# Plain float32 products for the DFTs, folds in place on VectorE, and the second sequence's transforms placed inside the first MoE

## What is computed

```python
batch, seq, dim = (2, 3008, 256)
X = np.fft.fft(x, axis=1)
X = np.fft.fft(X, axis=2).real          # attn_out
h = x @ w_in                            # 6016 x 256 @ 256 x 2048
g = h * (1.0 / (1.0 + np.exp(-h)))
x = g @ w_out
h = x @ w_in2
g = np.maximum(h, 0.0) + alpha * np.minimum(h, 0.0)
out = g @ w_out2
```

## Time and profile before

| | us |
|---|---|
| median of 3 runs | 1013.82 |
| lowest and highest | 1011.83, 1015.05 |
| the profiled execution, its own time | 1014.12 |
| its span, first to last instruction | 1012.3 |
| PE busy (4268 matmuls) | 969.5 |
| ACT, POOL, DVE busy | 590.4, 531.4, 452.8 |

### The profile page before, as it was taken

The page is one execution under the profiler, slowest core; times in us unless marked ns, Lnnn a source line. Parts: engine busy times, 40 slices in busy tenths (PEclk is TensorE's granted clock), DMA queues, the critical chain, the costliest instruction groups (busy, mean ns, idle before and its releaser), DMA issues.

```text
span 1012.3 us, 10975 instructions
## 1 busy us (share of the span) xinstructions
PE 969.5 (96%) x4268; PEld 807.8 (80%) x4268; DVE 452.8 (45%) x602; ACT 590.4 (58%) x708; POOL 531.4 (52%) x269
## 2 busy tenths in 40 slices
PE   3669999999999999999989999999999999999998
PEld 2568788888888888888878888888888888888887
DVE  7985785665554455545342322323223222322322
ACT  3426666666665566666656555555665565565554
POOL 5662955765555555555574544544444453444443
PEclk9869999999999999999999999999999999999999
DMA  8632200100000000000100000000000000000000
GB/s 285 236 119 63 84 22 11 52 31 12 21 1 9 13 1 1 1 0 1 29 14 21 1 21 20 1 21 1 21 21 1 21 0 21 1 21 21 1 21 20
DMA packets 13118, 31.93 MB, mean 32 GB/s; under 512 B 1373, under 2 KB 8841, under 8 KB 12041
## 3 DMA queue, kind: packets, MB, share of 16 engines
q1 hardware_dynamic: 12314, 24.29, 7.0%
q0 software_dynamic: 752, 6.94, 2.0%
HBM read 25.02 MB, written 6.21 MB: 31 GB/s over the span
## 4 chain that ended last, share of the span: by engine, by line
PE 89%; DVE 6%; POOL 2%; issue 1%; ACT 1%; DMA 0%; ACTq 0%; POOLq 0%; DVEq 0%
PE ps L341 13%; PE ps L343 13%; PE ps L342 13%; PE ps L564 8%; PE ps L601 8%; PE ps L607 8%; PE ps L560 8%; PE ps L602 8%; PE ps L561 8%; DVE fold_tmp L854 1%; POOL gl L1081 1%; DVE x_tile L841 1%; DVE g_sb L995 1%; POOL x_tile L1024 1%; DMA x_tile<-x_tiles 0%
## 5 line engine op out<-in xcount | busy, mean ns | idle before, releaser
L1081 POOL TENSOR_TENSOR gl<-g_sb,gh 128x1004 fp32r<-128x1004 f32 x192 | 416.7, 2170 | 431.4 <-ACT gh L750 276.9
L995 DVE SCALAR_TENSOR_TENSOR g_sb<-h_sb,neg_alpha,g_sb 128x502 f32<-128x502 f32 x192 | 157.6, 862 | 360.7 <-ACT g_sb L745 360.7
L750 ACT CAST gh<-g_sb 128x1004 fp32r<-128x1004 f32 x96 | 99.1, 1032 | 134.2 <-DVE g_sb L995 131.9
L971 DVE SCALAR_TENSOR_TENSOR h_sb<-n_all,a,v_sb 128x502 f32<-128x502 f32 x96 | 92.8, 966 | 168.4 <-ACT v_sb L782 165.5
L601 PE MATMUL ps<-gh,wo 128*128 128x502 f32 x384 | 149.8, 390 | 2.6 <-POOL wo L1006 2.6
L560 PE MATMUL ps<-gh,wo 128*128 128x502 f32 x384 | 149.1, 388 | 1.3 <-DVE pq L909 1.2
L343 PE MATMUL ps<-xs,wi 128*128 128x502 f32 x384 | 148.9, 388 | 0.0
L342 PE MATMUL ps<-xs,wi 128*128 128x502 f32 x384 | 148.7, 387 | 0.0
L341 PE MATMUL ps<-xs,wi 128*128 128x502 f32 x384 | 148.5, 387 | 0.0
L602 PE MATMUL ps<-gh,wo 128*128 128x502 f32 x384 | 148.1, 386 | 0.0
L561 PE MATMUL ps<-gh,wo 128*128 128x502 f32 x384 | 147.5, 384 | 0.0
(11 more groups left out here) (103 smaller groups left out, 1264.8 us busy)
## 6 DMA issues: line engine op xcount, KB each, us to landing
x_tile<-x_tiles SPq DMA_DIRECT2D x6, 1024.0 KB, 5.9
out_t<-out_sb SPq DMA_DIRECT2D x11, 502.0 KB, 2.8
stage<-moe_w_in SPq DMA_DIRECT2D x16, 256.0 KB, 3.8
stage<-moe_w_out SPq DMA_DIRECT2D x16, 256.0 KB, 2.8
n_parts<-n_rows SPq DMA_DIRECT2D x6, 502.0 KB, 3.5
t_sb<-t POOLq DMA_DIRECT2D x1, 2268.0 KB, 8.8
t_sb<-t POOLq DMA_DIRECT2D x3, 752.0 KB, 4.7
t_sb<-t POOLq DMA_DIRECT2D x1, 2256.0 KB, 9.5
```

The source lines that it names most:

```text
L995: ins = dve.scalar_tensor_tensor(out=gs[:, i, :], in0=m[:, i, :], scalar=neg_alpha[:, f:f + 1], in1=gs[:, i, :], op0=ALU.mult, op1=ALU.add)
L1081: pool.tensor_tensor(gl[g % 2][:, :, :], g_sb[g % 2][:, :, :], gh[g % 2][:, :, :].bitcast(F32), ALU.subtract).then_inc(gl_done, 1)
```

## The change

- **Plain float32.** All DFT products (feature and sequence) are single matmuls on float32 operands in place of `three`. `mt`, `w_sb`, the tables and the folded x are not split; `op_a` is gone (the matmul reads `xbuf`), `op_b` is written by the last fold. The MoE layers keep `three`.
- **Counts.** Before: 48 matmuls for the features, 96 for blocks 0 and 1, 90 for blocks 2, 3 and `n`. After: 16, 32 and 30.
- **Folds.** x is folded in place by DVE alone, nine instructions a tile (two sums, two even/odd, two halves, a small copy, two quarters). POOL does no arithmetic before `add_n(0)`.
- **Loads.** All table and x loads are issued by SP in one row, without waits; buffers are laid out so that none is shared. The tables are half as wide. The `a_line`, `a_rows` and first `n_rows`, `n_parts` DMAs move from SP to POOL.
- **Second sequence.** Its three tiles are folded in pieces by DVE, one piece after each of steps 2 to 22 of the first MoE. Its transforms are jobs on PE after steps 24, 25 (blocks 0, 1), 26, 27 (blocks 2, 3); the `n` products come after step 1. A job takes a turn of the two alternating pairs of banks. The `wi2` items move to every second step from 32 on.

```diff
+JOB_AFTER = {1: "n", 24: "t1p", 25: "t1q", 26: "t2", 27: "t3"}
...
+        TURNS = []
+        for g in range(STEPS):
+            TURNS.append(g)
+            if g in JOB_AFTER:
+                TURNS.append(JOB_AFTER[g])
...
+            elif former < STEPS1:
+                pe.wait_ge(h_done, former + 1)
...
-            STAGED_AT[NF + 2 + 2 * (i - WI2_ITEM)] = [i]
+            STAGED_AT[32 + 2 * (i - WI2_ITEM)] = [i]
...
+            def feature(fb):
+
+                if fb == 0:
+                    pe.wait_ge(mt_in, 16)
+                pe.wait_ge(w_in[fb], 16)
+                for m in range(2):
+                    for j in range(2):
+                        ins = pe.matmul(ps[:, 2 * fb + m, :], mt[:, j, m * P:(m + 1) * P],
+                                        w_sb[:, j, fb * 512:(fb + 1) * 512], start=j == 0, stop=j == 1)
+                    ins.then_inc(a_pe, 1)
...
+                    ins = pe.matmul(dst, xbuf[QT * b + q][rows, at:at + P], t1_sb[rows, 2 * q + r, :],
+                                    start=(q, r) == (blk, 0), stop=(q, r) == (blk + 1, 1))
...
+            def job(name):
+
+                turn_free(pe, name)
...
+                if 2 <= g < 23:
+                    fold_piece(QT + (g - 2) // 7, (g - 2) % 7)
...
+            pool.dma_start(eye2[0:NF, :], two_eye).then_inc(eye_in, 16)
+            pool.wait_ge(ab_lo, 8)
+            pool.dma_start(a_line, ab[0:1, 1, :, :].bitcast(F32)).then_inc(a_out, 16)
+            pool.wait_ge(a_out, 16)
+            pool.dma_start(a_rows[0:NF, :, :].bitcast(F32),
+                           a_line.rearrange("a i (f d) -> (a f) i d", d=P)).then_inc(a_in, 16)
+            pool.wait_ge(t1_lo, 2)
+            for i in range(2):
+                pool.dma_start(n_rows[0:1, i * N:(i + 1) * N], pq[0:1, 0, 2 + i, :].bitcast(F32)).then_inc(n0_out, 16)
+            pool.wait_ge(n0_out, 32)
+            pool.dma_start(n_parts[:, :, :].rearrange("p a t -> p (a t)"),
+                           n_rows[0:1, :].broadcast_to([P, 2 * N])).then_inc(n0_in, 16)
```

More of the change, by code:

```diff
@@ L145, in build @@
[L145 to L152, removed]
+        assert OPA_AT + 16320 + W2N * 2 <= W1_AT
@@ L173, in build @@
         stage_in = [sem(f"stage_in{i}") for i in range(SLOTS)]
+        stage_hi = sem("stage_hi")
+        stage_lo = sem("stage_lo")
+        mt_in = sem("mt_in")
+        w_in = [sem(f"w_in{i}") for i in range(4)]
         t1_in = [sem(f"t1_in{q}") for q in range(QT)]
@@ new lines, in _ @@
+            load_t1(1)
+            load_x(2)
+            load_t1(2)
+            sp.dma_start(t2_sb[:, :, :], t2).then_inc(t2_in, 16)
+            load_item(0)
+            sp.dma_start(t3_sb[:, :, :], t3).then_inc(t3_in, 16)
+            load_item(1)
+            load_x(3)
+            load_item(2)
+            load_item(3)
+            load_x(4)
+            load_x(5)
+            for i in range(4, WI2_ITEM):
+                load_item(i)
+            sp.wait_ge(t23_lo, t23_of(3, None, "n"))
@@ new lines, in transform23 @@
+            def transform23(blk, b, s):
+                sb, w = (t2_sb, BLOCK_W[2]) if blk == 2 else (t3_sb, BLOCK_W[3])
+                half = 1 if s == "q" else 0
+                dst = ps[0:72 if s == "n" else P, t_bank(blk, b, s), 0:w]
+                for q in range(QT):
+                    if s == "n":
+                        at0 = (3 - blk) * QT + q
+                        st = nop[:, at0:at0 + 72]
+                    else:
+                        st = op_b[QT * b + q][:, {2: (3, 0), 3: (1, 2)}[blk][half], :]
+                    ins = pe.matmul(dst, st, sb[:, q, half * w:(half + 1) * w], start=q == 0, stop=q == QT - 1)
+                ins.then_inc(t_pe, 1)
@@ new lines, in job @@
+            def job(name):
+                turn_free(pe, name)
+                if name == "n":
+                    pe.wait_ge(nop_ready, BATCH)
+                    transform23(2, None, "n")
+                    transform23(3, None, "n")
+                elif name in ("t1p", "t1q"):
+                    pe.wait_ge(fold, FOLDS * (NT - 1) + 7)
+                    for blk in range(2):
+                        for q in (blk, blk + 1):
+                            transform1(1, name[2], blk, q)
+                else:
+                    pe.wait_ge(fold, FOLDS * NT)
@@ L666, in job_dft_hi, with t1_copy @@
-            def job_dft_hi(blk, b, s):
-                job = job_of(blk, b, s)
-                act.wait_ge(job_pe, job + 1)
+            def t1_copy(b, s):
+                act.wait_ge(t_pe, t_pe_of(1, b, s))
+                if b:
+                    act.wait_ge(t1_sum, 2)
+                O = ps[:, t_bank(1, b, s), 0:T1W]
+                if s == "q":
+                    act.activation(o_sb[:, 2, :], O, ACT.Identity, scale=n_sign[:, 0:1])
+                act.copy(o_sb[:, "pq".index(s), :], O).then_inc(o_done, 1)
@@ new lines, in _ @@
+            act.wait_ge(spare_done, 1)
+            act.activation(spare[:, 0:1], spare[:, 1:2], ACT.Silu)
+            for fb in range(4):
+                for m in range(2):
+                    act.wait_ge(a_pe, 2 * fb + m + 1)
+                    act.copy(ab[:, m, 0, fb * 512:(fb + 1) * 512], ps[:, 2 * fb + m, :]).then_inc(ab_hi, 1)
+            act.wait_ge(sign_done, 1)
+            t1_copy(0, "p")
+            t1_copy(0, "q")
+            t1_round(0, "p")
+            t1_round(0, "q")
+            act.wait_ge(a2_pe, 1)
```

848 lines of the change are left out of this document (348 added, 500 removed).

## The result

The changed kernel took 984.54 us (median of 4 runs, 983.06 to 985.06) against 1014.17 of the kernel before (4 runs); the ratio is 0.971, 95% interval 0.969 to 0.973. The forecast was 993 with a range from 986 to 1007: right in direction and in part of its mechanism, 8.5 us too high, and 1.5 us outside the range.

A forecast was written before the change was run, and what follows sets the result against it. PE ends the chain nearly everywhere, after waiting for DVE in the prelude. Fifth step at 62.2 + 908.85 carried over + 19.3 for jobs + 1.2 beside POOL = 991.6 of span, so 993 us; range 986 to 1007.

The forecast's parts named there:

- The 908.85 carried unchanged: From the fifth MoE step's start to the span's end: all matmuls stay, so 908.85 us carry over.
- Jobs, 19.3: After steps 24 to 27 of the first MoE: 28 plain products, 19.3 us, in full on PE.
- The price of 0.69: A plain product of 376 columns on PE: four passes of 0.172 us at full clock, 0.69 us.
- The upper part of the bounds: Price of a plain product of 376 columns: up to 0.94 us, from three reduced products at the slow clock.
- the dear rival at 1.44: Rival: each pass of a plain product waits for its own weight load, 1.44 us a product: 1051 us; chance 0.09.
- The lock, 1.2: Steps 2 to 6 of the first MoE: DVE's fold pieces and POOL run serially on a shared port, 1.2 us.
- The waits of about a us for `gl` in steps 2 to 6: First MoE: sign expected if the forecast was right, PE waiting about a us for `gl`.
- The overload rival, up to 11 us: Rival: fold pieces overload DVE and POOL in the first MoE, up to 11 us: 1003 us; chance 0.11.
- Issues of POOL that DVE holds up, priced at 2 us: In the `n` chain: three DMA issues by POOL, each held up by a DVE instruction of 0.7, would add 2 us.
- The fifth step, 62.2: Prelude and first MoE steps: the fifth step starts at 62.2 us in place of 103.45, 41.3 earlier.
- The rival of late loads: Rival: x loads at 240 GB/s and 3 us more for the `n` chain: 998 us; chance 0.06.
- a cheap product alone: Rival: plain products at 0.52 us, 38 of them on the path save 6.5 us: 986.5 us; chance 0.04.

The follow-up runs named there:

- the experiment on the `n` chain: Changed kernel with the `n` row's stores and reload issued by SP instead of POOL, and POOL's first weight split put ahead of the `n` addition: 981.50 us.

## Why the prediction was nearly right, and what it missed

The sum was 62.2 + 908.85 + 19.3 + 1.2 = 991.6. What the trace has in its place is 66.1 + 899.2 + 16.0 + 1.7 = 983.0. The last three differences below nearly cancel (3.9 - 3.3 + 0.5 = +1.1), so the miss is that of the first.

- **The 908.85 carried unchanged: the step that failed, -9.6.** That the change "leaves all matmuls in it" is true, and their order is the same, but the diff also moved the buffers. The prediction took addresses to cost nothing and gave no case for it, up or down. What the runs show in its place: 8.0 us are the spacing, 1.6 the clock at the change of stage. From the third `gl` products to the last the kernel before takes 901.3 us. With four buffers moved it takes 893.3, with the same slow clock behind the wait of 2.6 us at the change of stage; with `gl` and `xs0` moved by 128 bytes it takes 891.7, at full clock there. The changed kernel takes 909.3, which is these 891.7 and the 17.7 put between. The clock behind that wait, with four buffers moved and with two:

```profile
515.00:517.00 2.00, 2.00 (x6) 1.57 (x5) 1.59 (x2) 0.89 (x2) 2.00 (x2) 0.50 0.00 0
```

```profile
514.00:516.00 2.00, 2.00 (x10) 1.68 (x9) 1.31 (x2) 1.16 (x2) 2.00 (x2) 1.00 0.00 0
```

  The wait of 2.6 us stands in 15 traces. PE was slow behind it in all six in which a buffer that PE streams was off the common rest, and in four of the nine others; the changed kernel's is one of the five fast ones, and has the highest mean clock of its four runs (0.997, the others 0.993 to 0.995). So most of the 1.6 us may be luck; that the change brings it is not shown.
- **Jobs, 19.3: -3.3.** They do lie in full on PE, as the prediction said. The price of 0.69 was the spacing of a reduced product, 0.172, times four. A plain product is 0.633 for 376 columns and was 0.857 for 512 in the feature products (0.92 predicted). The 136 further columns cost 0.224 us, 4 cycles of 2.4 GHz each, and 4 x 376 / 2400 = 0.627 leaves 6 ns beside the columns, where a reduced matmul has 15 (0.172 - 376 / 2400). The prediction charged these 15 four times. The upper part of the bounds, and the dear rival at 1.44, are out. The Trainium skill, FP8 and Floating Point Precision, TensorE Precision Notes, gives true float32 four passes; the trace agrees, with four cycles for each column.
- **The lock, 1.2: +0.5.** Measured 1.3 in the steps meant and 0.3 in the 16th, which the prediction did not have. The waits of about a us for `gl` in steps 2 to 6 are not there: five steps are each 0.1 to 0.3 us longer. The Trainium skill, SBUF — State Buffer, section on the two separate sides, has the port pair as an exclusive lock; the trace agrees: DVE's first `h` instruction took 1.67 us beside POOL's split and 0.74 where the split was moved. The overload rival, up to 11 us, is out: steps 7 to 22 but the 16th take 4.02 us with a fold piece in each. Issues of POOL that DVE holds up, priced at 2 us, are not seen: the two store issues took 0.5 us each in all traces with the chain on POOL, beside a DVE instruction or not.
- **The fifth step, 62.2: +3.9 in this execution.** PE started at 5.6 (5.0), DVE's folds began at 14.35 (12.9), and the releasing copy ended at 32.1 (30.5 was forecast); a fold took 4.9 (4.8). The last four products of block 1 stood behind a wait of 1.97 us and ran at the slow clock, 4.21 us for what took 2.77 in other executions; the prediction had PE arrive just in time there and priced no slow clock. The remainders ended at 40.8 in place of 38.0, the first step came at 41.24. The chain of `n` took 7.9 us to landing (7.1 forecast), and `h` 4.0 (3.2; POOL's split, not forecast at that place, is the difference). PE waited 4.6 (3.5 forecast), and the `n` products behind it were slow as forecast: 5.43 us. In the eight other executions of the same prelude that the experiment on the `n` chain lists, the fifth step came at 61.3 to 63.2, where the forecast had it, but that is in part luck. The waits and slow clocks that the forecast added up are not there: PE waited at most 0.6 us for `h_sb`, and the `n` products ran at full clock. In their place stand a wait of 2.0 to 3.9 us for the `a` row and the six products of block 2 behind it at the slow clock (5.7 to 7.1 us in place of 4.1), and the first step came at 42.0 to 44.5, not at 38.0.
- **The loads.** They came faster than any case had: 419 GB/s, where the earlier trace rows had 309, so the third x tile was never waited for. The rival of late loads is out. But the write of `a_line` behind them took 4.8 us to land and its reload 4.0, and PE waited 0.9 us for the `a` row here and up to 3.9 in the other traces, a wait no case had.

Faster by over 0.3% had 0.88, and it came. The mechanism held for the jobs and the lock, and for the fifth step in part; the stretch that was carried over did not hold. The range was too narrow on the fast side, since its lower end was set by a cheap product alone and no case let the old stretch shrink.

## What to carry to other kernels

When a change also moves buffers, a stretch that "stays the same" is not the same: compare the count of matmuls in 100 us between two profiles where PE is full, before any story on waits. Lay all operands that PE reads in turn at the same rest by 256 bytes, and measure it: here 128 bytes of offset on one small buffer cost about 8 us of 1000. Where a wait on PE is shortened, count what its end does to the clock: with block 1 late, the chain on SP gained 3.2 us of wait and 1.4 of clock. And look at several executions before a prelude is explained: here two of ten had the long wait, and the changed kernel's profile was one of them.

## What was not expected of the hardware

- Streaming one operand at another rest by 256 bytes than the others lengthens the spacing of the reduced matmuls of 502 columns, on the mean over all of them, from 0.2247 to 0.2269 us in the first MoE and from 0.2221 to 0.2240 in the second; it is PE's reading, not POOL's writing. The Trainium skill, SBUF — State Buffer, Operand start alignment, asks only for a multiple of the element size, and says that this is about legality and not speed; the runs agree, and show that speed asks for more.
- A plain float32 product costs four cycles a column and next to nothing more: 0.633 us for 376 columns at 2.4 GHz, while `three` costs 0.52. Products on 64 rows overlap when the lower and the upper half follow each other: 0.524 us on the mean of four whole and four half ones.
- Behind waits of 2 us PE came back at the slow clock in some executions and at the fast one in others, for the same instructions: 4.21 and 2.77 us for the last four products of block 1 behind a wait of 1.97, and 1.6 us more or less behind the wait of 2.6 at the change of stage.
